# A causal convolution moved from three engines to banded matrices on TensorE, with its rows kept in memory and the sums with U in rounded products

## The reference, cut to what matters

```python
# 1. convolution: 8 heads of 24 channels, 7 taps, weights normalized
w = exp(w - max(w)); w = w / (sum(w) + 1e-9)
x = einsum('hk,bskhg->bshg', w, windows of x padded with 6 zero rows in front)
# 2. first mixer: low rank over the rows, then two layers
h = x.transpose(0, 2, 1) @ U @ V          # U (S, 32), V (32, S)
u = x + h.transpose(0, 2, 1)
x = u + maximum(u @ w_ch1, 0) @ w_ch2     # 192 -> 768 -> 192
# 3. second mixer: Fourier transforms over rows and channels, real part
u = x + real(fft(fft(x, axis=1), axis=2))
un = (u - mean) / sqrt(var + 1e-6)
out = u + maximum(un @ w_ch1b, 0) @ w_ch2b
```

## Time and profile before

| | |
|---|---|
| median of 3 runs | 1343.79 us (1343.52 to 1348.24) |
| the profiled execution | 1343.88 us |
| its span, first to last instruction | 1341.6 us |
| mean granted clock of PE | 0.991 |
| DMA moved | 137.25 MB |

### The profile page before, as it was taken

One profiled execution on the slowest core, in us unless ns is written; L12 is line 12 of the kernel. 1 busy time (PEld: TensorE's weight loads), 2 busy tenths in 40 slices (PEclk: granted clock), 3 DMA queues, 4 the chain that ended last, 5 costly groups with the idle time before them and its releaser, 6 DMA issues.

```text
span 1341.6 us, 25362 instructions
## 1 busy us (share of the span) xinstructions
PE 1292.9 (96%) x9114; PEld 1250.9 (93%) x9114; DVE 952.2 (71%) x2417; ACT 724.2 (54%) x1772; POOL 477.7 (36%) x630
## 2 busy tenths in 40 slices
PE   7799997999999999999999999999999999999998
PEld 7599886899999999989999999999999999999998
DVE  8778897568867868855786886965656666655554
ACT  5256664445557656634555665744444655555553
POOL 0123563123533545621132474651101244433332
PEclk9899999999999999999999999999999999999999
DMA  9843212422244642113224323211223223222220
GB/s 272 293 139 111 86 55 84 120 101 93 97 166 155 194 144 90 49 43 109 79 65 145 105 81 127 77 40 49 78 63 100 66 86 98 87 70 80 81 80 36
DMA packets 62510, 137.25 MB, mean 102 GB/s; under 512 B 8836, under 2 KB 24844, under 8 KB 60327
## 3 DMA queue, kind: packets, MB, share of 16 engines
q1 hardware_dynamic: 58354, 129.22, 30.3%
q0 software_dynamic: 4032, 6.41, 1.5%
HBM read 89.67 MB, written 51.49 MB: 105 GB/s over the span
## 4 chain that ended last, share of the span: by engine, by line
PE 79%; DVE 14%; DMA 2%; issue 2%; ACT 1%; POOL 1%; SPq 0%; POOLq 0%; ACTq 0%; DVEq 0%
PE bank L617 17%; PE bank L618 7%; PE bank L598 7%; PE bank L606 6%; PE bank L605 6%; PE bank L602 6%; PE bank L599 6%; DVE X L1085 5%; PE bank L651 4%; PE bank L621 3%; PE bank L678 2%; DVE ht L997 2%; PE bank L669 2%; PE bank L668 2%; DVE X L1131 2%
## 5 line engine op out<-in xcount | busy, mean ns | idle before, releaser
L804 ACT ACTIVATE ht<-bank 128x384 fp32r<-128x384 f32 x528 | 259.8, 492 | 467.1 <-PE bank L606 459.2
L997 DVE SCALAR_TENSOR_TENSOR ht<-bank,ht 128x384 fp32r<-128x384 f32 x528 | 293.0, 555 | 280.2 <-ACT ht L804 278.0
L617 PE MATMUL bank<-w,ht 128*128 128x384 f32 x1320 | 418.7, 366 | 9.0 <-DVE ub L1005 8.2
L618 PE MATMUL bank<-w,ht 128*128 128x192 f32 x1320 | 331.6, 251 | 0.0
L1219 POOL TENSOR_TENSOR ub<-ub,tmp 128x576 f32<-128x576 f32 x88 | 125.9, 1430 | 461.2 <-DVE ub L1005 329.1
L617 PEld LDWEIGHTS bank<-w,ht 128*128 128x128 f32 x1320 | 249.2, 189 | 16.7 <-issue 10.0
L618 PEld LDWEIGHTS bank<-w,ht 128*128 128x128 f32 x1320 | 252.9, 192 | 0.0
L598 PE MATMUL bank<-uth,w1h 128*128 128x384 f32 x528 | 189.1, 358 | 0.5 <-ACT uth L794 0.4
L1085 DVE SCALAR_TENSOR_TENSOR X<-xin,cw,X 128x264 f32<-128x264 f32 (+2 forms) x300 | 179.0, 621 | 5.0 <-ACT X L873 3.3
L602 PE MATMUL bank<-utl,w1h 128*128 128x384 f32 x528 | 179.7, 340 | 2.1 <-DVE utl L1022 2.1
L605 PE MATMUL bank<-uts,w1s 128*128 128x384 f32 x528 | 179.8, 341 | 0.8
(11 more groups left out here) (115 smaller groups left out, 2533.5 us busy)
## 6 DMA issues: line engine op xcount, KB each, us to landing
f1t<-f_copy SPq DMA_DIRECT2D x44, 396.0 KB, 3.2
x_two<-ub SPq DMA_DIRECT2D x44, 288.0 KB
ub<-x_two SPq DMA_DIRECT2D x44, 288.0 KB, 3.1
mix<-mixed SPq DMA_DIRECT2D x44, 288.0 KB, 3.3
out<-ub SPq DMA_DIRECT2D x44, 288.0 KB
vch<-v_split SPq DMA_DIRECT2D x44, 192.0 KB, 2.8
mixed<-rowk SPq DMA_DIRECT2D x88, 74.2 KB
xin<-in_x SPq DMA_DIRECT2D x4, 1632.0 KB
```

What stands on the lines that cost most here:

```text
L617: e.matmul(dn[t][:, 0:2 * D], hh, w2[ph][:, m, :], start=(m == 0), stop=False)
L618: mm = e.matmul(dn[t][:, 0:D], hl, w2[ph][:, m, 0:D], start=False, stop=False)
L804: e.activation(hth[q % 4], up[q % 3][:, 0:TOK], ACT.Relu).then_inc(act_h, 1)
L997: e.scalar_tensor_tensor(htl[q % 4], up[q % 3][:, 0:TOK], 0.0, hth[q % 4].bitcast(F32), ALU.max, ALU.subtract).then_inc(dve_l, 1)
```

## The change

**Tiles of 122 rows.** The host lays out x anew before the launch: 35 tiles of 128 rows that overlap by 6, so that each gives CT = 122 convolved rows. The last tile is moved back to the end of the batch, and its first 46 rows are computed twice and left out. U is laid out in the same tiles (with zeros in those rows), and V by columns of the blocks.

**Convolution on PE.** From the normalized taps DVE builds one row per head with the seven taps in a field of zeros, ACT's queue stores it, and loads it back as 128 shifted rows; reversed, this is a banded 128x122 matrix per head. `convolve` multiplies it with 24 channels of nine tiles (eight in the last of the four pieces) in plain float32. Two heads share a bank. Batch 0 is convolved ahead of the loop in six banks, the others at eight places each, four heads at a place, in both banks `tb`: batch 1 in blocks 1 to 8, batch 2 in blocks 11 and 20 to 25, batch 3 in blocks 34 to 41.

**Evacuation.** ACT copies each pair out over x's own rows and rounds it into `xhl`; POOL (DVE for half of batch 0, with DVE taking the low parts there) subtracts for the low part.

**Memory.** The convolved rows are stored in a tensor `x_conv`, and each block of phase 0 loads its rows into its slot of `ub`, two blocks ahead; X and `LATE` are gone. `part_of_t` multiplies [U high, U low] (64 columns) with [x' high, x' low] (384 columns) in one rounded matmul per tile, 35 a batch; DVE adds the four quarters.

```diff
+CT = N1 - PAD
+NT = -(-S // CT)
+PW = 9
+PIECES = [(p, min(PW, NT - p)) for p in range(0, NT, PW)]
+V_PARTS = [(0, 12), (12, 23), (23, N2)]
...
             if c == 2:
+                spots = [(n0, 1), (n0 + 9, 1), (n0 + 10, 1), (n1, 1), (n1 + 1, 1), (n1 + 1, 3), (n1 + 2, 3), (n1 + 3, 1)]
...
             else:
+                spots = [(n0 + k, 1) for k in range(1, 9)]
+                stores = [(n0 + k, 3) for k in (2, 4, 6, 8)]
+                loads = [(n0 - NB + 2, 5), (n0 - NB + 4, 1), (n0 + 3, 1), (n0 + 5, 1)]
+                parts = [(n0 + k, 5) for k in (2, 4, 6, 8)]
+                t_last[(n0 + 9, 1)] = c
+            for k, (n, m) in enumerate(spots):
+                p, first = k // 2, k % 2 * 2
+                conv[(n, m)] = [(c, p, first), (c, p, first + 1)]
+                high_at[(n, m + 1)] = low_at[(n, m + 2)] = conv[(n, m)]
...
              # SP, ahead of the loop
+            va = V_PARTS[0][1] * 128
+            for n in range(4):
+                e.dma_start(vraw[n * R:(n + 1) * R, 0:va], V[:, 0:va]).then_inc(ld_v[0], 16)
+            e.dma_start(u_raw[:], U).then_inc(ld_u, 16)
+            for p, (j0, w) in enumerate(PIECES):
+                e.dma_start(xin0[:, j0:j0 + w, :], x[0, :, j0:j0 + w, :]).then_inc(ld_x[p], 16)
...
             store_v(0)
+            load_w1(0, w1a)
+            store_x(0, 0)
+            load_w2(0, w2a)
+            store_x(0, 1)
+            store_x(0, 2)
+            e.wait_ge(v_stored[0], 16)
             load_v(0)
             load_v(1)
+            store_x(0, 3)
+            load_u(0)
+            load_u(1)
+            for n in range(4):
+                e.dma_start(vraw[n * R:(n + 1) * R, va:], V[:, va:]).then_inc(ld_v[1], 16)
+            e.dma_start(f1d[:, 0:2], f1[:, 0:2]).then_inc(ld_f1, 16)
+            load_x(1, 0)
             e.wait_ge(ld_f1, 16)
             load_f1(0)
             load_f1(1)
+            e.dma_start(f1d[:, 2:], f1[:, 2:]).then_inc(ld_f1, 16)
+            load_x(1, 1)
+            e.dma_start(mir[:], mirror).then_inc(ld_mir, 16)
+            load_w1(1, w1b)
+            for to, source in ((lowd, low), (highd, high), (bcd, bc)):
+                e.dma_start(to, source).then_inc(ld_tab, 16)
             load_v(2)
...
             def part_of_t(c, p):
+                for j in range(w):
+                    mm = e.matmul(o[0:2 * R, 0:2 * D], uhl[:, j0 + j, :], src[0:CT, j].rearrange("p a d -> p (a d)"),
+                                  start=(j == 0), stop=(j == w - 1))
...
+            def convolve(c, p, k):
...
+                for h in range(2):
+                    mm = e.matmul(o[0:CT, 0:w * 2 * HD].rearrange("p (t c) -> p t c", c=2 * HD)[:, :, h * HD:(h + 1) * HD],
+                                  band[:, 2 * k + h, :], src[:, :, (2 * k + h) * HD:(2 * k + h + 1) * HD],
+                                  start=True, stop=True, skip_group_check=True)
...
+            def convolved(c, p, k):     # ACT
+                bk, q = full(e, ("conv", c, p, k))
+                copy(tiles_of_pair(xin[p % 2], p, k), bank_of_pair(bk, p)).then_inc(tb_free[q], 1)
...
             def make_u(n):              # DVE
+                e.wait_ge(u_in[n % UR], (n // UR + 1) * 16)
```

More of the change, by code:

```diff
@@ L29 @@
 EPS = 1e-6
[L30 to L41, removed]
+CT = N1 - PAD
+NT = -(-S // CT)
+TAIL = S - CT
+OVER = (NT - 1) * CT - TAIL
+PW = 9
+PIECES = [(p, min(PW, NT - p)) for p in range(0, NT, PW)]
+NP = len(PIECES)
+PAIRS = H // 2
+FILLS = NP * PAIRS
+QW = 250
+V_PARTS = [(0, 12), (12, 23), (23, N2)]
 PUT_OFF = 8
-RING = 3
 ROWS = 3
@@ L122, in program @@
         zs = sb("zs", [128, 2 * KC, N2], F32R)
[L123 to L127, removed]
+        xin = [sb(f"xin{n + 1}", [128, PW, D], F32) for n in range(2)]
+        xhl = sb("xhl", [128, PW, 2, D], F32R)
+        band = sb("band", [128, H, CT], F32)
         f1t = sb("f1t", [128, 2, 2, TB, 2 * KC], F32R)
         vch = sb("vch", [4 * R, 2, TB, 128], F32R)
-        u_sb = sb("u_sb", [128, N2, R], F32)
+        uhl = sb("uhl", [CT, NT, 2 * R], F32R)
         def split(name, shape):
@@ L301, in fill_both @@
             fill((kind, n, 1), 1, act)
-        fill(("t", 0, 0), 0, False)
+        for p in range(NP):
+            fill(("t", 0, p), p % 2, False)
         fill_both("low", 0, False)
@@ L308, in program @@
             for m in range(M6):
-                if m == 0 and nx is not None and phase(nx) == 0 and n != LATE:
+                if m == 0 and nx is not None and phase(nx) == 0:
                     fill_both("low", nx, False)
@@ L312, in program @@
                     fill((kind, b, g), q, True)
-                if m == 2 and nx is not None and n != LATE:
+                for q, piece in enumerate(conv.get((n, m), ())):
+                    fill(("conv",) + piece, q, False)
+                if m == 2 and nx is not None:
                     fill_both("turn", nx, True)
@@ L374, in taken, with pieces_out, x_stored, pair_of @@
             e.wait_ge(tb_free[q], k + 1)
[L378 to L401, removed]
+        def pieces_out(c, p):
+            return c * 32 + (p // 2 + 1) * 16 if p % 2 == 0 else c * 48 + (16 if p < NP - 1 else 48)
+        def x_stored(e, c):
+            e.wait_ge(x_out[0], pieces_out(c, NP - 2))
+            e.wait_ge(x_out[1], pieces_out(c, NP - 1))
+        def pair_of(c, p, k):
+            return c * FILLS + p * PAIRS + k
         def x2_free(e, n, how):
@@ L508, in store_u, with load_u @@
+            def load_u(n):
+                ph, b, i = blocks[n]
+                u_free(e, n)
+                if i == 0:
+                    x_stored(e, b)
+                pattern = [[N2 * D, 128], [D, TB], [1, D]]
+                e.dma_start(u_slot(n), bass.AP(xc.tensor, b * (S * D) + i * (TB * D), pattern)).then_inc(u_in[n % UR], 16)
             def store_u(n):
@@ L763, in _ @@
                         up_slot(n, m + 2)
-                    elif nx is not None and n != LATE:
+                    elif nx is not None:
                         if m == 4 and phase(nx) == 1:
@@ L774, in _ @@
                             group_out(b, g)
-                    if m == 2 and nx is not None and n != LATE:
+                    for piece in conv.get((n, m), ()):
+                        convolve(*piece)
+                    if m == 2 and nx is not None:
                         turn(nx)
@@ L914, in diagonal @@
-            def diagonal(h):
-                for k in range(K):
-                    e.activation(diag[:, h - DIAG_0, k, :], ident[:], ACT.Copy, scale=cw[:, h, k:k + 1]).then_inc(act_dg, 1)
-            def conv_evacuate(n):
-                e.wait_ge(pe_cv, n + 1)
-                j0, w = PIECES_0[n]
-                for half in range(2):
-                    first = H - 2 * (half + 1)
-                    skip = max(VEC_HEADS_0[n] - first, 0)
-                    c = slice((first + skip) * HD, (first + 2) * HD)
-                    src = CONV_BANKS[n][half][:, 0:w * 2 * HD].rearrange("p (t c) -> p t c", c=2 * HD)[:, :, skip * HD:]
-                    cp = copy(X[:, j0:j0 + w, c], src)
-                cp.then_inc(act_cv, 1)
@@ new lines, in _, with v_high @@
+            e.dma_start(taps.rearrange("(o h) q -> o (h q)", o=1), tap_row[:].rearrange("p h q -> p (h q)")).then_inc(taps_out, 16)
+            def v_high(n):
+                a, z = (v * 128 for v in V_PARTS[n])
+                e.wait_ge(ld_v[min(n, 1)], 64)
+                copy(ht[0:4 * R, 0:z] if n == 0 else vlate[:, a - V_PARTS[1][0] * 128:z - V_PARTS[1][0] * 128],
+                     vraw[:, a:z]).then_inc(v_h, 1)
+            v_high(0)
+            e.wait_ge(taps_out, 16)
+            e.dma_start(steep[:], bass.AP(taps.tensor, 0, [[1, 128], [QW, H], [1, CT]])).then_inc(steep_in, 16)
@@ L968, in _ @@
                             group_q(b, g)
+                    for piece in conv.get((n, m), ()):
+                        convolved(*piece)
+                    for piece in high_at.get((n, m), ()):
+                        convolved_high(*piece)
                     if m == 1 and pv is not None and phase(pv) == 0:
                         x2_high(pv)
-                    if m == 2 and nx is not None and n != LATE:
+                    if m == 2 and nx is not None:
                         turned_high(nx)
@@ L1221, in add_mixed @@
             def add_mixed(n):
-                e.wait_ge(xm_in[n % UR], (sum(phase(k) == 1 for k in range(n % UR, n, UR)) + 1) * 16)
+                e.wait_ge(u_in[n % UR], (n // UR + 1) * 16)
                 e.wait_ge(mix_in, (count(n) + 1) * 16)
```

520 lines of the change are left out of this document (232 added, 288 removed).

## The result

The changed kernel takes 1448.95 us (median of 4 runs, 1447.96 to 1454.19), against 1346.01 for the kernel before on the same chips. The ratio is 1.077, with a 95% interval of 1.073 to 1.081. I had predicted 1329 us, in a range of 1305 to 1348, and gave a slower kernel 0.12. It is slower by 103 us, so the direction was wrong too.

The account below looks back on a forecast made before the run. PE was taken as the bound: 1343.9 + 6.5 (start) - 46.4 (convolution off the other engines) + 19.8 (added PE work) + 5 (banks) = 1328.8, predicted 1329 us, range 1305 to 1348.

Parts of the forecast that it names:

- What bounds the kernel now: PE, busy 96%; against a floor of PE work per stage, 46.4 us are lost where DVE, ACT and POOL convolve.
- I take the whole 46.4 us as gone: Blocks 1 to 54: moving the convolution off DVE, ACT and POOL gains the whole loss; bounds 35 and 46.4 us.
- Cost on PE: Loop: convolution adds 11.7 us a batch, sums fall from 11.4 to 6.3; net 19.8 us for three batches.
- Banks: Pairs of heads take both shared banks at 24 places in the loop: 0.2 us each, 5 us in all; bounds 0 and 26.
- Rival (3): At 24 places PE waits for two evacuations and a rounding: 40 us instead of 5, total 1364 us; chance 0.10.
- Memory in the loop: Convolved rows stored and loaded back, 3.2 MB a batch each way: costed at nothing, loads having about 6 us of lead.
- The start: Ahead of the third block's low-rank product: 23.1 MB on SP's queue at 279 GB/s puts it at 85 us, losing 6.5.
- The band at "about 20": In the start, the banded tap weights are ready for PE at about 20 us, while x is still landing.
- The two trips "of 2.5 to 3": In the start, tap weights go to memory and back as a band, each trip taking 2.5 to 3 us.
- The 1.8 us: Possible extra for the band's load in 488-byte pieces, under the 512-byte limit; the sum would then read 1331.
- The sum: Whole kernel: the profiled time plus and minus the priced terms gives 1328.8, predicted 1329 us.
- Rival (2): A later start, from 768-byte rows, the band behind x and the low clock: point at 96, total 1340 us; chance 0.13.

Follow-up runs that it names:

- experiment 1: Changed kernel with the stores of convolved rows and the load of U each split into 112 and 10 partitions: 1334.57 us, ratio to before 0.993.
- experiment 5: Kernel of experiment 1 with each banded product inside the loop done twice, same result: 1371.31 us (one run).
- experiment 3: Changed kernel with stores still on 122 partitions, but each partition's piece written as one long run instead of rows of 768 bytes: 1436.52 us (one run).
- experiment 4: Split U load kept, stores of convolved rows cut differently from experiment 1: 61 and 61 partitions 1694.44 us, 120 and 2 partitions 1340.27 us.
- experiment 7: Experiment 1 with its queue reordered, f1 copied in three: 1313.59 us; also holding the rest of x until the band landed: 1305.39 us.

## Why the prediction was wrong

**What bounds the kernel now: right, up to 5 us in one stage.** In the repaired kernel of experiment 1 blocks 2 to 6 take 15.72 and 14.71 us by turns, as the adds that close blocks 3, 4 and 5 show:

```profile
136.91 1.43 POOL L1228 TENSOR_TENSOR ub<-ub,tmp 128x576 f32<-128x576 f32 x1 [6.12 <-DVE ub L1032]
152.63 1.43 POOL L1228 TENSOR_TENSOR ub<-ub,tmp 128x576 f32<-128x576 f32 x1 [7.41 <-DVE ub L1032]
167.34 1.43 POOL L1228 TENSOR_TENSOR ub<-ub,tmp 128x576 f32<-128x576 f32 x1 [6.12 <-DVE ub L1032]
```

Two of them are 30.43, and the floor is 2 x 12.98 + 2 x 1.46 + 1.57 = 30.45. So the loss put down to the convolution on DVE, ACT and POOL (28.9 us in blocks 1 to 10; 28.6, if the stage is counted from 78.9 as the others are) is gone whole there, as the step "I take the whole 46.4 us as gone" had it. Blocks 44 to 54, from which the convolution has moved out, went from 169.4 to 157.0, where the floor without their share of T is 157.1.

**Cost on PE: right.** The products run 8 records in 1.46 us, 0.183 each (0.187 taken); a sum of nine matmuls takes 1.57, 0.174 each (0.18 taken). From the chain of experiment 1:

```profile
138.73 1.46 PE bank L751 x8
149.35 1.57 PE bank L735 x9
```

The changed kernel and that of experiment 1 show it in blocks 33 to 43: 159.9 instead of 147.1, where 8 x 1.46 + 4 x 1.5 - 3.8 = 13.9 of work came and a loss of 0.8 went.

**Banks: the size near, the place not.** I took 0.2 us at each of 24 places, 5 us. Blocks 2 to 6 and 33 to 43 show none of it. But the stage of blocks 22 to 32 takes 183.0 us in experiment 1 against a floor of 178 (173.6 - 7.6 + 5 x 1.46 + 3 x 1.57), so some 5 us are lost there, where two DFTs stand beside the products. The list of waits has 1.9 us there, none of it for a copy out of a bank; what takes the rest, and whether it is new or a remnant of the 10.6 us that I took as gone in this stage, stays open. That the 5 us fit the sum is luck. Rival (3), 40 us of waits for evacuations, is out by the list in experiment 5.

**Memory in the loop: the step that failed.** "I cost it at nothing" rested on the mean share of the DMA engines and on 3.1 us to landing of a tile of 128 partitions. The new stores have 122, and none of the rows before showed such a transfer, so the landing of another shape was no price for it. I should have kept both ends: 128 partitions on one side, a single engine on the other. In the changed kernel these stores ran on 2 of 16 engines, about 18 us for 0.84 MB, and held what stood behind them on SP. That cost 47 us in the loop (3.5 + 13.6 + 30.1).

**The start: the same error.** The sum of bytes over 279 GB/s gave 85 us for the third block's low-rank product. It came at 154.6: 3.24 MB of stores went out at 47 GB/s, and small loads of V stood behind them. Up to the end of block 0 this cost 66 us against experiment 1. With the transfers recut it came at 88.96, so the sum of bytes was right for a queue that uses all engines, 4 us short. The band at "about 20" was off as well: 34 us in the changed kernel (U on two engines until 23), 26 in the recut one. The two trips "of 2.5 to 3" took 6.0 and 16.05 us there, and with x held back 5.9 and 3.60. The 1.8 us set beside the sum for its pieces of 488 bytes can't be told from these runs.

**The sum.** With the transfers recut, as in experiment 1, 1334.6 was measured against the forecast of 1329: +4 for the start and 2 for the rest. None of my rivals had the mechanism. Rival (2) named the store's rows of 768 bytes, and priced them at 11 us; what experiment 3 gives for long rows on two engines is 12, but the factor of eight in the number of engines was not in any case I wrote down.

## What to carry to other kernels

Before a tile size other than 128 goes through DMA, factor the partition count: what counts, by the rule cited in Theory A and by the runs at 122 and 61, is its largest divisor up to 16. Cut an awkward count into a multiple of 16 and a rest, as the 112 and 10 here. A mean DMA share hides such a transfer, since 2 engines that are full all the time showed as 0.14 here: look for stretches where everything waits and the share is a constant small fraction. And where one queue issues everything, check the order by deadline, since one slow store holds up every small load behind it.

## What the runs showed of the hardware

- One DMA engine moved 23 to 24 GB/s in rows of 768 bytes (47 on two from 77 to 94 us of the changed kernel, 23 on one in experiment 4), and 27 to 28 in rows of 6.9 and 5.4 KB (55 on two from 81 to 94 us in experiment 3).
- Behind a store of 1098 rows of 768 bytes on two engines, the issuing queue itself stood: the issue of a load of 128 partitions took 15.2 us. Behind the same bytes in 122 rows it took 0.4 (experiment 3).
- Transfers of two queues share the engines unevenly: the same load of 488-byte pieces took 16.05 us beside the load of x (experiment 1) and 3.60 with three of x's four pieces held back (experiment 7), which is 139 GB/s.
- PE's granted clock was 0.50, its lower level of 1.2 GHz, from 77 to 94 us of the changed kernel, where PE had been idle since the sums of batch 0, at 55.9.
